# Attention and two gated layers on one core: the first group's head pairs in one order, with other query transfers and idle products

## The reference

```python
kv = np.einsum('bhsd,bhse->bhde', k, v)
out = np.einsum('bhsd,bhde->bhse', q, kv)
rms = np.sqrt(np.mean(out * out, axis=-1, keepdims=True) + 1e-06)
x = (out / rms * g_norm)              # to (2304 tokens, 512)
h = x @ w_in                          # 512 -> 2048
x = (h * sigmoid(h)) @ w_out          # 2048 -> 512
x = ((x @ w_a) * (x @ w_b)) @ w_out2  # 512 -> 1536 -> 512
```

## Time and profile before

| | us |
|---|---|
| median of 3 runs | 870.26 |
| lowest, highest | 870.24, 873.62 |
| the profiled execution's own time | 873.04 |
| its span (first to last instruction) | 871.2 |
| TensorE busy in the span | 860.4 (99%) |
| GpSimd, VectorE, ScalarE busy | 610.1, 510.6, 279.0 |

### The profile page before, as it was taken

One profiled execution on the slowest core, in us unless ns is written; L12 is line 12 of the kernel. 1 busy time (PEld: TensorE's weight loads), 2 busy tenths in 40 slices (PEclk: granted clock), 3 DMA queues, 4 the chain that ended last, 5 costly groups with the idle time before them and its releaser, 6 DMA issues.

```text
span 871.2 us, 16097 instructions
## 1 busy us (share of the span) xinstructions
PE 860.4 (99%) x6208; PEld 813.8 (93%) x6208; DVE 510.6 (59%) x776; ACT 279.0 (32%) x465; POOL 610.1 (70%) x889
## 2 busy tenths in 40 slices
PE   8899999999999999999999999999999999999998
PEld 5699999999999999999999999999999999999997
DVE  4665656757886666665765355364484553544636
ACT  3764434534543323222532122121242211212210
POOL 2566545666578777766778697797889876877760
PEclk9999999999999999999999999999999999999999
DMA  9664123111011111111101111021011330210104
GB/s 300 158 156 106 49 57 75 50 49 49 26 49 49 46 28 50 50 49 49 49 25 49 50 49 49 25 63 60 25 49 49 109 98 25 74 49 25 49 25 109
DMA packets 47002, 55.56 MB, mean 64 GB/s; under 512 B 11728, under 2 KB 32464, under 8 KB 46928
## 3 DMA queue, kind: packets, MB, share of 16 engines
q1 hardware_dynamic: 44192, 49.55, 19.9%
q10 hardware_dynamic: 2736, 4.98, 1.8%
HBM read 49.81 MB, written 4.72 MB: 63 GB/s over the span
## 4 chain that ended last, share of the span: by engine, by line
PE 98%; DVE 1%; issue 1%; ACT 0%; POOL 0%; POOLq 0%
PE ps L777 49%; PE ps L863 8%; PE ps L864 8%; PE ps L865 8%; PE ps L885 6%; PE ps L887 6%; PE ps L886 6%; PE ps L794 3%; PE ps L737 2%; PE ps L747 1%; PE ps L989 1%; PE ps L709 1%; PE ps L723 1%; DVE o_sb L1350 0%; DVE stat L1331 0%
## 5 line engine op out<-in xcount | busy, mean ns | idle before, releaser
L777 PE MATMUL ps<-x_hi,w_hi 128*128 128x288 f32 x1064 | 229.8, 297 | 0.5 <-issue 0.3
L777 PE MATMUL ps<-x_lo,w_hi 128*128 128x288 f32 x1064 | 228.1, 296 | 0.0
L777 PE MATMUL ps<-x_hi,w_lo 128*128 128x288 f32 x1064 | 226.8, 295 | 0.0
L777 PEld LDWEIGHTS ps<-x_hi,w_hi 128*128 128x128 f32 x1064 | 179.0, 188 | 13.7 <-issue 5.1
L777 PEld LDWEIGHTS ps<-x_hi,w_lo 128*128 128x128 f32 x1064 | 171.7, 189 | 0.0
L777 PEld LDWEIGHTS ps<-x_lo,w_hi 128*128 128x128 f32 x1064 | 169.9, 188 | 0.0
L1142 ACT COPY kept<-ps 128x576 f32<-128x576 f32 x114 | 73.2, 642 | 288.1 <-PE ps L777 287.6
L523 POOL TENSOR_SCALAR w_hi<-wt 128x256 fp32r<-128x256 f32 x152 | 69.9, 460 | 123.4 <-PE ps L777 116.4
L1473 DVE TENSOR_TENSOR xy<-xy,ps 128x384 f32<-128x384 f32 (+1 forms) x188 | 94.0, 510 | 89.0 <-PE ps L865 88.7
L863 PE MATMUL ps<-g_hi,d_hi 128*128 128x384 f32 x384 | 129.0, 336 | 0.2
L864 PE MATMUL ps<-g_lo,d_hi 128*128 128x384 f32 x384 | 128.9, 336 | 0.0
(11 more groups left out here) (111 smaller groups left out, 1236.7 us busy)
## 6 DMA issues: line engine op xcount, KB each, us to landing
raw<-in_moe_w_out_dram SPq DMA_DIRECT2D x28, 512.0 KB, 3.6
raw<-in_moe_w_in_dram SPq DMA_DIRECT2D x15, 512.0 KB, 3.5
raw<-in_moe_w_a_dram SPq DMA_DIRECT2D x12, 512.0 KB, 3.5
raw<-in_moe_w_b_dram SPq DMA_DIRECT2D x12, 512.0 KB, 3.5
kvq<-in_k_dram SPq DMA_DIRECT2D x8, 576.0 KB, 5.5
out_dram<-xy SPq DMA_DIRECT2D x26, 128.0 KB, 2.4
kvq<-in_v_dram ACTq DMA_DIRECT2D x4, 576.0 KB, 11.4
kvq<-in_v_dram SPq DMA_DIRECT2D x4, 576.0 KB, 5.9
```

Source lines behind the costliest of these rows:

```text
L777: mm = pe.matmul(ps[:, bank + s, 0:PART], w, x[:, n, c, s * PART:(s + 1) * PART], start=(begins and first), stop=last, skip_group_check=no ...
```

## The change

- The query loads of group 0 are divided by head and no longer by batch. SP loads the even head of a pair and ScalarE's queue the odd one. Each covers all 128 partitions: 64 rows of batch 0 and 64 of batch 1, with one head's 576 values in each.
- SP waits, besides for the last queries, for the fourth `kv` before it issues the second group's first loads.
- Idle products: eight and eight of 128 columns, the identity by the identity, in place of three and two of 512 columns of zeros. VectorE's clear of `wt` and the wait for it go.
- Pair 0 loses its exception: results of pair 0 are turned and kept in turn with pair 1's `q_kv`, and VectorE's query copies of pair 1 alternate with the normalises of pair 0, on all of TensorE, ScalarE and VectorE.

```diff
-    WARM = (3, 2)
+    WARM = (8, 8)
...
-        def queries(h, bb):
-
-            dst = kvq[h][bb * HALF:(bb + 1) * HALF, 2, :].rearrange("p (h e) -> p h e", h=2)
-            return dst, q[bb, 2 * h:2 * h + 2].rearrange("h (p t) d -> p h (t d)", t=ROWS)
+        def queries(h, odd):
+
+            return (kvq[h][:, 2, odd * SEQ:(odd + 1) * SEQ],
+                    q[0:2, 2 * h + odd].rearrange("b (p t) d -> b p (t d)", t=ROWS))
...
             sp.wait_ge(q_in[PAIRS - 1], 32)
+            sp.wait_ge(kv_mm, PAIRS)
             load_heads(0)
...
             def warm(count):
                 for _ in range(count):
-
-                    zeros = wt[:, 0:2, :].rearrange("p a n -> p (a n)")
-                    pe.matmul(ps[:, first_bank(1, 0), :], ident[:], zeros, start=True, stop=True)
+                    pe.matmul(ps[:, first_bank(1, 0), 0:P], ident[:], ident[:], start=True, stop=True)
 
             pe.wait_ge(consts, 3)
-            pe.wait_ge(cleared, 1)
...
                 for j in range(JS):
-                    if h > 1:
+                    if h:
                         o_turn(0, h - 1, j, result_bank(h - 1, j))
                     q_kv(0, h, j, prod_bank(h, j))
                 if h + 1 < PAIRS:
 
                     kv(0, h + 1)
                     for j in range(JS):
-                        if h == 0:
-
-                            o_turn(0, 0, j, result_bank(0, j))
                         q_turn(0, h + 1, j, first_bank(h + 1, j))
...
-                    if h > 1:
+                    if h:
                         keep(0, h - 1, j, result_bank(h - 1, j))
...
-                if h == 0:
-                    for j in range(JS):
-                        keep(0, 0, j, result_bank(0, j))
...
-            nc.vector.memset(wt[:, 0:2, :], 0.0).then_inc(cleared, 1)
             nc.vector.memset(kv_sb[:], 0.0).then_inc(cleared, 1)
-            dve.wait_ge(cleared, 2)
+            dve.wait_ge(cleared, 1)
...
                     normalise(0, h, j)
-                    if 0 < h < PAIRS - 1:
+                    if h < PAIRS - 1:
                         qT_keep(0, h + 1, j, first_bank(h + 1, j))
-                if h == 0:
-
-                    for j in range(JS):
-                        qT_keep(0, 1, j, first_bank(1, j))
```

More of the change, by code:

```diff
@@ L1069, in kv_keep @@
                     act.wait_ge(o_mm, JS * (n - 1))
-                act.wait_ge(cleared, 2)
+                act.wait_ge(cleared, 1)
                 for odd, bank in enumerate((BANK_D, BANK_D + 1)):
```

## The result

| | before | after |
|---|---|---|
| median | 870.25 (870.21 to 873.62, 4 runs) | 907.25 (906.63 to 909.63, 4 runs) |
| the profiled execution's own time | 873.04 | 906.63 |
| its span | 871.2 | 904.8 |

All in us. The ratio of after to before is 1.0419, with a 95% interval of 1.0395 to 1.0443: slower, by 37.0 us of the medians and 33.6 us of the spans. The forecast was 903 us, with a range of 866 to 917.

What follows compares the result with a forecast made beforehand. TensorE, busy 99%, bounds the kernel, so time moves with `plain(0)`, held by query transfers. +32.5 us and three zero terms on 873.04 give 905.5, less 2.8 for that execution's excess over the median: 903 us, range 866 to 917.

Steps and rivals of the forecast that it cites:

- The two engines: Query transfers by head: a source with two batches outermost is shared by two DMA engines instead of 16.
- The landing: Last queries of group 0 land at 63.7 us instead of 26.7, 37.0 us later.
- After the landing: From first query transpose at 64.2 us to `plain(0)`, the first layer's first product, 6.8 us: `plain(0)` at 71.0.
- The sum: `plain(0)` +32.5 us, and 0 each for the second group's loads, the pair order and the idle products: 903 us.
- rival 1: Query transfers keep 16 engines: `plain(0)` at 35.2 to 37.7 us, gain 0.8 to 3.3 us, 868 us; chance 0.22.
- The later loads of the second group: SP issues the second group's loads 37 us later, its new wait costing nothing: cost 0, up to 1 us on GpSimd.
- The idle products: TensorE's first eight take 3.7 us, then a 1.7 us pause and 1.3 us more for `kv`: hidden, cost 0.
- The order: One order for all pairs frees some 2 us of pair 1, hidden behind its wait for data: cost 0.
- Rival 3: Two engines and ACT's issuing stalls: ACT starts near 45 to 48 us, `plain(0)` near 77, 909 us; chance 0.14.
- that `kv` is done near 53 us: The fourth `kv`, for which SP newly waits, is done near 53 us, ahead of the queries at 63.7.
- only the last pair counts: Pairs' queries come some 15 us apart and a pair's own chain took 8 us, so earlier pairs add nothing.
- one of its signs: The DMA share falls to a tenth or two from about 15 to 62 us.

Runs made afterwards that it cites:

- Experiments 1 to 3: The change with queries by batch (869.62 us); the kernel before with queries by head (907.66 us); the change with each head's load split per batch (870.09 us).
- experiment 6: The change with queries loaded by batch and without SP's wait for the fourth `kv`: 869.39 us, ratio 0.9974 to the kernel before.
- experiment 2: The kernel before with only the query loads divided by head: 907.66 us, ratio 1.0418.
- experiment 5: The change with head pairs 0 and 1 loaded by batch and only pairs 2 and 3 by head: 887.3 us, ratio 1.0187.

## Why the prediction was right

**The two engines.** The step on which the forecast stood was "I take two". It was an inference from the shape of the source. Experiments 1 to 3 and the packet counts show it: the loss is there with the two-batch transfers whatever else is changed, and gone when the same pieces go in transfers whose source has 64 rows outermost.

**The landing.** Forecast 63.7 us, from 1440 KB on each engine at 24.1 GB/s; GpSimd started on them at 65.28. The rate came from a window in which all sixteen engines worked; that it holds for two alone was not known. The spacing of the pairs was forecast as 15 us and was 16.2, 15.3 and 14.3.

**After the landing.** Forecast 6.8 us from the first transpose to `plain(0)`, between 5.1 and 8.1; it was 6.19 (65.85 to 72.04), with the transposes at the half clock (2.18 us) and most of the rest not. GpSimd's side was ready early enough, if only just: its first two rests ended at 71.01 (forecast 69.1), TensorE was there at 72.04. The w_in half was late by the 0.37 us in its row.

**The sum.** +32.5 us for `plain(0)`; measured +33.55, and +33.6 in the span. The forecast for the median was 4.2 us too low, and the larger part of that is no term of the sum. I took 2.8 us off because the profiled execution of before lay that far above its median. The profiled execution of after lies 0.6 us below its own. So the medians differ by 37.0 us, 3.4 more than the spans. Larger samples of the kernel before have medians of 871.75, 871.85 and 872.21, nearer to its profiled time, and against these the change costs some 35 us; from the first three runs this was not to be seen. The range is no test of the forecast: it reached down to 866 for rival 1, so that it would have held the kernel without any loss too.

**What was called hidden.** The later loads of the second group: SP issued them at 65.25 us, and the span moved by no more than `plain(0)`. The fourth `kv` ended at 61.1, 8 us later than I wrote, still ahead of the queries; experiment 6 shows that SP's wait is free without that cover too. The idle products: the first set took 3.79 us (forecast 3.7), and the first `kv` then ran at the low clock, 2.20 us in place of 1.29. The order: with late queries 0.75 us at most, by experiment 2.

**Rival 3 was half right, and the forecast left its stall out.** The issuing stalled and ScalarE started at 40.77 us, 4 to 7 us ahead of the 45 to 48 named. Three pairs of some 6 us each did follow (18.4 us together, to 61.1), but the last queries were still 24 us away when ScalarE started, so the three pairs ended 4.2 us ahead of them and `plain(0)` was not held until 77. That the stall is hidden is thus a matter of 4 us: on this side the forecast had some luck. Against it I had said that "by 7 us ACT had issued all without a visible stall", but the earlier trace rows are of a kernel in which sixteen engines share the load, and say nothing of two full ones. The forecast's own "that `kv` is done near 53 us" and "only the last pair counts" took no account of it. Nor did one of its signs come: the DMA share was to fall to a tenth or two from 15 us, and was 0.40 from 25 to 35 us, since k and v of the later pairs were issued so late. Of the kernel before the prediction says that the DMA engines are nearly full over the first slices; in the earlier trace rows only the first slice has a 9, and the next two have a 6.

**Rival 1** is what the other edits do when the queries are not late. It was given 868 us; its two kernels measured 869.62 and 869.39 where before stood at 871.75 and 872.21. Its reading of the 2.26 us, a wait for an instruction block whose place goes with the number of instructions, is borne out by the table above.

## What to carry to other kernels

Ask of every transfer what its outermost dimension is on both sides, in the form in which it is issued. An edit that moves the same bytes in the same pieces, over more partitions, put them on 2 engines in place of 16 because "two batches" had become the outermost dimension of the source; a split into one transfer per batch undid that here (870.09 us against 907.25). When a DMA share settles at a tenth or so while somebody waits for data, divide its GB/s by what one engine moves at full load: that gives the number of engines, here 52 by some 25. And compare the count of small packets with that of a kernel that differs in these transfers alone.

## What the runs showed of the hardware that was not expected

- An issuing queue waits when the engines that it feeds are behind: single issues of 12.84 and 11.83 us on ScalarE's queue, and on SP's as well (before, then after):

```profile
3.40 1.29 SPq L479 DMA_DIRECT2D gcol<-in_g_norm_dram  x2
5.49 14.12 SPq L479 DMA_DIRECT2D gcol<-in_g_norm_dram  x2
```

These are two transfers of 64 values each, so what they wait for must be the ones ahead of them, an inference that no row shows by itself. The issues of k and v of the third and fourth pair, which sixteen engines share, stood in the same two queues behind such waits; that of v in ScalarE's queue took 12.84 and 11.83 us.
- One engine moved at most 26 GB/s when two carried the load (52 GB/s in all, in the stretch shown above), and 24.7 by the spacing of the pairs in experiment 5. With all sixteen loaded it was 24.1 in the best stretch of the earlier trace rows, and from 2.5 to 16 us 22.0 in before (352 GB/s) and 19.9 in experiment 5 (318 GB/s). A sum over bytes per engine needs the rate for its own stretch.
- A pause of TensorE between instructions with nothing to wait for was 0.85 to 2.26 us long while the transfers ran. The Trainium skill, "Runtime: NRT & Kernel Launch", section "Instruction fetch mechanics", calls the fetch of an instruction block mostly hidden; the pauses behind 449 and 705 instructions, which end 1.3 to 1.65 us behind a block's transfer, speak against it under a full DMA load. Where the load was light it was hidden: in the change TensorE passed 449 and 705 at 48.47 and 54.45 us without a stop. No run varies the fetch by itself.
